# The product with the values, head by head: 64 stationary and 64 moving columns in place of 128 by 128

## The reference

```python
scores = scale * np.matmul(q, k.transpose(0, 1, 3, 2))
mask = (rel >= 0) & (rel < window)          # window = 64
scores = np.where(mask, scores, -1000000000.0)
scores = scores - np.max(scores, axis=-1, keepdims=True)
attn = np.exp(scores)
attn = attn / (np.sum(attn, axis=-1, keepdims=True) + 1e-09)
attn_out = np.matmul(attn, v)
x = attn_out.transpose(0, 2, 1, 3).reshape(B * S, H * D)
h = x @ w_in;   x = np.maximum(0.01 * h, h) @ w_out      # layer 1
h = x @ w_in2;  out = (h * np.cos(h)) @ w_out2           # layer 2
```

## Time and profile before

| | |
|---|---|
| time, median of 3 runs | 911.75 us (911.4 to 912.96) |
| span of the profiled execution | 910.0 us |
| PE busy | 891.0 us (98%) |
| PE weight loads busy | 846.9 us (93%) |
| DVE busy | 477.5 us (52%) |
| ACT busy | 393.2 us (43%) |
| POOL busy | 83.9 us (9%) |
| granted TensorE clock, whole span | 1.00 (2.4 GHz) |

### The profile page before, as it was taken

One profiled execution on the slowest core, in us unless ns is written; L12 is line 12 of the kernel. 1 busy time (PEld: TensorE's weight loads), 2 busy tenths in 40 slices (PEclk: granted clock), 3 DMA queues, 4 the chain that ended last, 5 costly groups with the idle time before them and its releaser, 6 DMA issues.

```text
span 910.0 us, 14462 instructions
## 1 busy us (share of the span) xinstructions
PE 891.0 (98%) x5040; PEld 846.9 (93%) x5040; DVE 477.5 (52%) x1146; ACT 393.2 (43%) x978; POOL 83.9 (9%) x68
## 2 busy tenths in 40 slices
PE   6799999999999999999999999999999999999998
PEld 5799999999999999999999889998999999999997
DVE  6755555545555554555323555545545545545543
ACT  5566444433433343434345534434433434434433
POOL 2254300000000000000256400000000000000000
PEclk9999999999999999999999999999999999999999
DMA  8455322222221222220444300100200100100100
GB/s 279 136 168 177 113 77 64 64 84 63 63 71 64 76 63 73 60 67 0 142 116 139 116 1 0 69 0 0 69 0 0 69 0 0 69 0 0 36 1 36
DMA packets 36878, 59.72 MB, mean 66 GB/s; under 512 B 3952, under 2 KB 24816, under 8 KB 36848
## 3 DMA queue, kind: packets, MB, share of 16 engines
q1 hardware_dynamic: 36848, 59.33, 21.0%
HBM read 49.87 MB, written 9.44 MB: 65 GB/s over the span
## 4 chain that ended last, share of the span: by engine, by line
PE 94%; DVE 3%; ACT 1%; issue 1%; DMA 0%; SPq 0%; ACTq 0%; DVEq 0%
PE h_ps L305 43%; PE y_ps L330 22%; PE y_ps L337 21%; PE s_ps L265 3%; PE t_ps L292 3%; PE t_ps L280 1%; DVE probs L564 1%; DVE x_raw L577 1%; DMA qk_sb<-qk 0%; DVE probs L539 0%; DVE neg_max L546 0%; DVE row_sum L552 0%; ACT w_hi L400 0%; DVE act_in L598 0%; DVE probs L596 0%
## 5 line engine op out<-in xcount | busy, mean ns | idle before, releaser
L305 PE MATMUL h_ps<-x_hi,w_hi 128*128 128x384 f32 x768 | 264.0, 344 | 1.1 <-DVE g_raw L604 0.6
L305 PE MATMUL h_ps<-x_lo,w_hi 128*128 128x384 f32 x768 | 258.3, 336 | 0.0
L305 PE MATMUL h_ps<-x_hi,w_lo 128*128 128x384 f32 x768 | 257.6, 335 | 0.0
L305 PEld LDWEIGHTS h_ps<-x_hi,w_hi 128*128 128x128 f32 x768 | 144.7, 188 | 5.9 <-DVE g_raw L604 1.0
L305 PEld LDWEIGHTS h_ps<-x_hi,w_lo 128*128 128x128 f32 x768 | 144.5, 188 | 3.7
L305 PEld LDWEIGHTS h_ps<-x_lo,w_hi 128*128 128x128 f32 x768 | 144.2, 188 | 0.3 <-DVE x_lo L583 0.3
L610 DVE TENSOR_TENSOR g_lo<-g_raw,g_hi 128x384 fp32r<-128x384 f32 x192 | 107.2, 558 | 68.4 <-ACT g_hi L448 68.4
L448 ACT ACTIVATE g_hi<-g_raw 128x384 fp32r<-128x384 f32 x192 | 100.7, 524 | 93.9 <-DVE g_raw L604 56.1
L589 DVE TENSOR_TENSOR g_raw<-h_ps,act_in 128x384 f32<-128x384 f32 x96 | 53.5, 557 | 164.4 <-ACT act_in L430 164.4
L330 PE MATMUL y_ps<-g_hi,w_hi 128*128 128x384 f32 x384 | 134.1, 349 | 0.0
L430 ACT ACTIVATE act_in<-h_ps 128x384 f32<-128x384 f32 x96 | 47.1, 490 | 194.4 <-PE h_ps L305 194.4
(11 more groups left out here) (43 smaller groups left out, 961.0 us busy)
## 6 DMA issues: line engine op xcount, KB each, us to landing
qk_sb<-qk SPq DMA_DIRECT2D x72, 224.0 KB, 2.6
v_sb<-values SPq DMA_DIRECT2D x72, 128.0 KB, 2.1
w_raw<-w_in SPq DMA_DIRECT2D x32, 256.0 KB, 2.7
w_raw<-w_out SPq DMA_DIRECT2D x32, 256.0 KB, 2.9
layer_out<-y_out SPq DMA_DIRECT2D x6, 768.0 KB, 3.8
x_raw<-layer_out SPq DMA_DIRECT2D x6, 768.0 KB, 5.2
out<-y_out SPq DMA_DIRECT2D x5, 768.0 KB, 4.0
mask_sb<-mask SPq DMA_DIRECT2D x18, 128.0 KB, 2.1
```

Source lines behind the costliest of these rows:

```text
L305: mm = pe.matmul(h_ps[j % 2][:, 0:CH], w[:, j, cols], x[:, kt, :], start=kt == 0 and a == 0, stop=kt == KT - 1 and a == 2)
```

## The change

`values` issues four matmuls for a unit in place of two: for each tile a and each head h, 64 stationary columns (the head's features) and 64 moving columns (the head's queries), over the same 128 keys. Head h writes PSUM partitions 64h to 64h+63, columns 64a to 64a+63, so the result stands as `x_raw` wants it. `copy_o` is then one copy of 128 partitions x 128 elements. Waits and semaphores are as they were: `pv_done` is raised once by the last matmul, `o_copied` once by the copy.

```diff
                 for a in range(2):
-                    mm = pe.matmul(o[:, P * a:P * a + P], v[:, P * a:P * a + P], probsT[:, p % 2, P * a:P * a + P],
-                                   start=True, stop=True)
+                    for h in range(2):
+                        head = slice(P * a + D * h, P * a + D * h + D)
+                        mm = pe.matmul(o[D * h:D * h + D, TILE * a:TILE * a + TILE], v[:, head],
+                                       probsT[:, p % 2, head], start=True, stop=True)
                 mm.then_inc(pv_done, 1)
...
                 o = banks[2][p % len(banks[2])]
-                for h in range(2):
-                    head = slice(D * h, D * h + D)
-                    o_h = o[head, 0:2 * P].rearrange("p (a h q) -> p a h q", a=2, h=2)[:, :, h, :]
-                    x_h = x_raw[head, hp, P * i:P * i + P].rearrange("p (a q) -> p a q", a=2)
-                    last = dve.tensor_copy(x_h, o_h)
-                last.then_inc(o_copied, 1)
+                dve.tensor_copy(x_raw[:, hp, P * i:P * i + P], o[:, 0:P]).then_inc(o_copied, 1)
```

## The result

The changed kernel takes 924.91 us (median of 4 runs, 923.98 to 925.94) against 911.64 us before: ratio 1.0138, 95% interval 1.0126 to 1.0150. It is slower by 13.3 us (the difference of the two medians; the ratio gives 12.6). The forecast was 920.8 us, so the direction and the range (902 to 938) held, and the middle was 4.1 us short.

What follows compares the result with a forecast made beforehand. PE was taken to bound the chunks and VectorE the prologue: +10.0 us for the product in 60 units and -1.0 us in the prologue make +9.0, 911.75 to about 920.8 us, range 902 to 938.

Steps and rivals of the forecast that it cites:

- The bound: From 46 to 430 us PE never waits, so whatever it gains or loses per unit moves the end by as much.
- The product: Four narrow matmuls for two wide ones in a full PE: +0.166 us per unit, +10.0 us over 60 units.
- records that go by width: In the product, eight narrow records take 0.444 us, exactly what four wide ones take: change 0.
- the two bare weight loads: At each unit's two switches of shape, loads not hidden behind a matmul: 0.055 + 0.111 = 0.166 us per unit.
- the switches: Changes of matmul shape into and out of each narrow group: forecast 0.166 us per unit, between 0 and 0.49.
- the drain of the rival: Rival: each switch of shape empties the array, 29.4 us, total 940; chance 0.28 together with a fixed price per record.
- the full price of 0.49: Upper bound per unit for both switches: bared pipeline depth 0.161 and 0.163 us plus loads of 0.055 and 0.111.
- My own sign for the forecast: Timeline distance from the first narrow record to the scores, 0.45 us before, should become 0.50 to 0.73 us.
- The overlap rival: Rival: the two heads' records run at once on array halves, up to 0.222 us gained per unit, 897 us; chance 0.17.
- free switches: Condition for the overlap's full gain: changing matmul shape costs nothing, so each unit gains up to 0.222 us.
- My objection: Against overlap in the product: a float32 matmul is two records on the same half, so only neighbours can pair.
- The copy: One VectorE copy of 0.285 us for two of 0.57: worth 0 in the chunks, 1.2 us in the prologue.

Runs made afterwards that it cites:

- the half of the array: Changed kernel with all narrow matmuls writing PSUM partitions 0 to 63 and two copies of 64 partitions, against the kernel before: 935.75 us, ratio 1.0255.
- head order: Changed kernel with its four narrow matmuls reordered, both tiles of head 0 and then both of head 1, against the kernel before: 925.82 us, ratio 1.0152.
- the copy alone: Kernel before with its wide product kept and one copy of 128 partitions in place of two: 914.45 us, ratio 1.0028.

## Why the prediction was right, and what in it was not

**The bound.** Right. PE is busy for all of 46 to 430 us, and what a unit costs PE appears in the time 60 times over. The table shows nothing else between the prologue and chunk 5, j = 2; only 0.26 us follow at the start of chunk 5.

**The product: the sum was right, its two terms were not.** The forecast was "records that go by width" with no overlap, 0, plus the two bare weight loads, 0.166 us. Measured is 0.162 us per unit. But it is made of -0.213 for the overlap (-0.227 against the half of the array), which I had as a rival with a chance of 0.17 and as a lower bound of -0.222, and of 0.375 for the switches, which I had at 0.166 with an upper bound of 0.49. Two errors of 0.2 us cancelled: that the forecast's middle fits per unit is luck. The bare loads were sized well as far as the timeline can split them: of the scores' 0.47 us, 0.11 is more than before. What was left out is that PE also waits before the first load of the other shape: 0.10 us on entry, and about 0.15 us between the group's last start and the scores' first (0.38 - 0.23) where records of that shape follow each other at 0.05 to 0.06. This is the drain of the rival, at 0.10 us per edge in place of the 0.16 that the whole pipeline depth would have been. By the Trainium skill's rule, "TensorEngine Tiling (Array Packing)", section Key Properties, a change of tiling mode drains TensorE: the trace agrees, with 0.375 us for a pair, three quarters of the full price of 0.49.

My own sign for the forecast, a distance of 0.50 to 0.73 us from the first narrow record to the scores, failed: it is 0.38. I had put the entry's price inside that distance, but most of it lies ahead of the first record, and the exit's load inside the scores. Someone who had looked at this distance alone would have called the kernel faster. The distance from the down matmul ahead to the up matmul behind is the one that counts.

**The overlap rival.** Its mechanism was right (for it: 0.23 us for eight records, 0.46 on one half), its condition ("free switches") was not. The Trainium skill's "TensorE: Matmul & The Clock Gate", section Part 3, on concurrent column tiles, agrees. My objection, that two records of one float32 matmul share a half so that only neighbours pair, was wrong: even in head order the group takes 0.39 us.

**The copy.** 0.285 us expected, 0.284 measured, and worth nothing in the chunks, as said. In the prologue I expected 1.2 us for the copy and lost 0.2 to the product; the copy alone gives 1.3 us in its trace, the changed kernel in its own only 0.3. The prologue scatters by more than that: the same mark came 1.2 us sooner with two copies and the narrow product, 3.1 us with the order of the heads, and from 1.3 sooner to 0.2 later in five kernels with the same prologue. Neither the 1.2 nor the 0.2 us is confirmed one by one; the change in the prologue as a whole gave 2.2 us by the medians, against the 1.0 of the forecast. (A normalisation that is not stretched takes 0.44 us, not the 0.42 that I wrote; nothing hangs on it.)

**The missing term.** 4.1 of the 13.3 us are the stop of VectorE at the second layer's loop. I wrote "DMAs, semaphores and buffers are the same" and that after 430 us nothing changes; the code's length changed, by 36 instructions ahead of that loop. I also wrote that the change brings no idle time that would put the clock in doubt; the stop brought it, and about 1.6 of the 4.1 us fall in the stretch at the lower clock behind it. Without the stop the kernel takes 920.9 us, where I forecast 920.8. That closeness is luck too, as the terms above show.

## What to carry to other kernels

Narrow matmuls on two halves of the array do run beside each other, but a group of them between full-width matmuls pays 0.375 us for its two edges, with eight records as with sixteen: eight lose, sixteen just win, so gather them until the gain (0.213 us for every eight records here) is well above the edges, or use them where PE has time to spare. Measure such a change from the last instruction ahead of the group to the first behind the next, never inside it. And when a change makes an engine's program shorter or longer, look at the entries of its loops for time in which the engine waits for nothing: 4 us of this kernel's loss had nothing to do with the product, and part of it was the clock that fell behind the wait.

## What the runs showed that I had not expected

- **The prologue's granted clock.** In the trace before it was 1.00. In the changed kernel it was half (1.2 GHz) from 28.4 to 35.2 us; from 26 to 30 us PE was busy for 1.67 of 4.00 us:

```profile
26.00:30.00 4.00, 1.67 (x16) 1.03 (x18) 3.61 (x12) 2.28 (x9) 1.47 (x2) 0.80 0.48 138
30.00:34.00 4.00, 4.00 (x32) 3.42 (x30) 1.90 (x5) 1.27 (x4) 1.28 (x1) 0.50 0.93 282
```

  The kernel before was busy for only 1.22 us of the stretch from 26 to 30 us and kept its clock, and with the copy alone the clock fell too (0.93 over 10 to 35.5 us). The change is not needed for it. The kernel before with 92 VectorE instructions more has the same prologue as the kernel before, and its clock was half from 21 to 27.7 us:

```profile
21.00:27.70 6.70, 5.89 (x24) 5.60 (x25) 6.50 (x22) 4.48 (x15) 3.40 (x3) 0.50 0.58 174
```

  There it cost nothing that shows (the mark at the prologue's end is at 36.2 us against 36.1), since VectorE was busy for 6.50 of the 6.70 us. In the changed kernel the fall lies later, where PE is busy for 4.00 of 4.00 us, and may have taken back part of VectorE's gain; that was not tried. What makes the clock fall at one place in one execution and not in another is open.
- **PE pairs records across four places of its program** (head order, 0.39 against 0.38 us for the group).
- **An engine's stop of 5.9 us without a releaser** that comes and goes with 36 instructions, stays away with 92 more, and is followed by a lower clock of another engine.
